# Routing code copied into both branches on the limits, with the flag read before the bias is built

## The chip, the cores and the metric

The kernel runs on one core of a Trainium2 chip. Its time is the device time of one launch in microseconds, and each time given for a kernel is the median of several runs. Engines are TensorE (PE; PEld is its weight load), VectorE (DVE), ScalarE (ACT), GpSimd (POOL) and SyncE (SP), which issues most DMA transfers here. An engine name with a q (PEq, DVEq) is that engine's sequencer, which reads registers, branches and waits.

## The reference

Local attention with a few global keys, then a mixture of 8 experts with one expert per token, then a dense mixture of 4 experts:

```
scores = scale * q @ k.T + bias(n_global, n_local)      # B=2, H=8, S=768, D=64
attn   = softmax(where(keep, scores, -1e9)) @ v         # n_global=8, n_local=96
x      = attn reshaped to [1536, 512]
xn, en = x / |x|, expert_emb / |expert_emb|
logits = xn @ en.T / tau;  idx = argmax(logits);  gate = softmax(logits)[idx]
out    = gate * (relu(x @ w1[idx]) @ w2[idx])           # 8 experts, 512 -> 1024 -> 512
p      = domain_probs / sum
result = sum_e p[:, e] * (relu(out @ v1[e]) @ v2[e])    # 4 experts, all tokens
```

`n_global` and `n_local` are inputs of the program, so the kernel doesn't know them when it is built.

## The kernel before

Each engine runs its own program, and semaphores order them. At the start DVE turns the two limits into a flag `flag_i` (L619 to L625): 1 if the limits are small enough for a windowed attention, 0 if a general one must be used. Every engine but GpSimd reads that flag into a register (`flag_of`, L347) and branches with `If(fast > 0)` ... `Else()`. With the inputs of this case the flag is 1, and the fast branch runs. The general branch is long on DVE and on TensorE (24 unrolled heads and tiles in a loop body), and in the program it lies between the fast branch and what follows both.

In the fast branch attention runs as a pipeline over 4 pairs of heads (`hp`), each with 12 tiles of 128 queries (`i`). `pipeline` writes pair 0 out, loops over pairs 1 and 2, and writes pair 3 out again. For each tile TensorE makes the scores (L1006), DVE adds the bias and takes the row maximum (L703), ACT takes the exponential (L527), TensorE transposes (L1018), ACT copies (L535), TensorE multiplies by the values (L1032), ACT copies (L542), TensorE turns the result (L1046) and DVE normalises it (L738, L740). Beside pair 0 some set-up steps run once: `scale_embeddings` (L643 to L647, of which L645 scales the 8x512 embeddings), `turn_embeddings` on TensorE (L987) and `keep_embeddings` (L654 to L659). `squares` (L680 on DVE, L513 on ACT) sums the squares of each finished tile during the last pair.

Before the pipeline DVE squares the embeddings (L628), waits for the constants (`const_ready`) and builds the bias with six operations (L633 to L638). It reads the flag after these. TensorE runs `keep_busy(32)`, 32 matmuls on a constant tile whose result is never used (L977), waits for the identity matrix (`ident_ready`) and then reads the flag; another `keep_busy(24)` stands between the scores of tile 0 and of tile 1. GpSimd from early on splits weights in two parts (L272 copies the high part, L277 subtracts it for the low part), a quarter of a unit at a time, as the quarters land from DMA.

After the branches comes the routing. On DVE L835 to L887: logits, norms (waiting for `norm_ready` from ACT's root, L519), the maximum, the one-hot table (L849), the ranks that TensorE counts (L1100, L1102), the position of each token (`pos_i`, L866), the tables of slots (up to L881), and the gates (L884 to L887), for which ACT takes one exponential (L561). GpSimd then scatters 12 tiles of tokens to DRAM by `pos_i` (L472). TensorE waits for 8 of them, runs `keep_busy(40)`, and starts the experts with the first gathered tile (L1123); DVE's first step there is L896. The lines that matter most:

```
dve.wait_ge(x_written, HP * DUO)
...
route(nc.vector.tensor_tensor(rt[:, 1], lg[:, 0], lg[:, 1], ALU.add))
...
def flag_of(eng):
    eng.wait_ge(flag_ready, 1)
    return eng.value_load(flag_i[0:1, 0:1], min_val=0, max_val=1)
```

Of the kernel before, what the change touches and what calls it, by code (L numbers as in the profile page):

```python
# [51 lines left out]
def fused_kernel(nc, qkv, limits, emb, tau, probs, wts, consts, out):  # L52
# [6 lines left out]
    with ExitStack() as ctx:  # L59
# [439 lines left out]
        def _(act):  # L499
# [20 lines left out]

            fast = flag_of(act)
            with act.If(fast > 0):
# [23 lines left out]
                norms()  # L546
            with act.Else():
                act.wait_ge(bias_built, 1)
# [60 lines left out]
        def _(dve):  # L609
            done = [0]  # L610

            def step(ins, s=setup_step):
# [14 lines left out]
            dve.wait_ge(emb_ready, 16)  # L627
            nc.vector.tensor_tensor_reduce(out=embq_t, in0=emb_t, in1=emb_t, scale=1.0, scalar=0.0,  # L628
                                           op0=ALU.mult, op1=ALU.add, accum_out=norm_e[:, 0:1]).then_inc(emb_sq, 1)
# [4 lines left out]
            step(nc.vector.scalar_tensor_tensor(mask_t, key_t, ng, mask_t, ALU.is_lt, ALU.max))  # L634
            nc.vector.tensor_scalar(slope_t, rel_t, nl, -0.5 / SCALE, ALU.min, ALU.mult)
            step(nc.vector.tensor_scalar(mask_t, mask_t, -1.0, 64e9 / SCALE, ALU.add, ALU.mult))
            nc.vector.tensor_tensor(bias[:, 0, :], slope_t, mask_t, ALU.add)
            nc.vector.scalar_tensor_tensor(bias[:, 1, :], slope_t, 0.5, mask_t, ALU.mult, ALU.add).then_inc(bias_built, 1)  # L638
            dve.wait_ge(bias_built, 1)
# [9 lines left out]
            def keep_embeddings(idle_times=2):  # L649
# [33 lines left out]

            before_paths = done[0]
            fast = flag_of(dve)
            with dve.If(fast > 0):
                def await_scores(hp, i):


                    n = hp * DUO + i  # L690
                    dve.wait_ge(scores_ready, n + 1)
                    if started(n - 1):
                        dve.wait_ge(transposed, n - 1)
                    if i < 3 and not isinstance(hp, int):
                        dve.wait_ge(bias_ready, 2 * hp if i == 2 else 2 * hp - 1)
# [35 lines left out]
                def normalise(hp, i):  # L731
# [5 lines left out]
                    for hh in range(2):  # L737
# [88 lines left out]
            dve.wait_ge(x_written, HP * DUO)  # L826
            done[0] = 0

            def route(ins):
                step(ins, route_step)  # L830

            def wide(x):
                return x.to_broadcast([P, NT, E])

            route(nc.vector.tensor_tensor(rt[:, 1], lg[:, 0], lg[:, 1], ALU.add))  # L835

            dve.wait_ge(norm_ready, 1)
            route(nc.vector.tensor_scalar(rs[:, 2], rs[:, 1], 1e-6, tau_sb[:, 0:1], ALU.add, ALU.mult))
            route(nc.vector.reciprocal(rs[:, 3], rs[:, 2]))
            route(nc.vector.tensor_tensor(rt[:, 0], rt[:, 1], wide(rs[:, 3]), ALU.mult))  # L840
            route(nc.vector.tensor_reduce(rs[:, 4, :, 0], rt[:, 0], AX.X, ALU.max))
            nc.vector.tensor_tensor(rt[:, 1], rt[:, 0], wide(rs[:, 4]), ALU.subtract).then_inc(shifted_ready, 1)
            dve.wait_ge(shifted_ready, 1)

            route(nc.vector.scalar_tensor_tensor(rt[:, 3], rt[:, 1], 0.0,
                                                 rank8.rearrange("p (a e) -> p a e", a=1).to_broadcast([P, NT, E]),
                                                 ALU.is_ge, ALU.mult))
            route(nc.vector.tensor_reduce(rs[:, 5, :, 0], rt[:, 3], AX.X, ALU.max))
            nc.vector.tensor_tensor(onehot[:, 0:NT, :], rt[:, 3], wide(rs[:, 5]), ALU.is_equal).then_inc(onehot_ready, 1)  # L849


            dve.wait_ge(ranks_ready, 1)
            rank = ps[:, 3, 0:(NT + 1) * E].rearrange("p (t e) -> p t e", e=E)
            route(nc.vector.tensor_scalar(cnt_i[:, 0, :], rank[:, NT, :], float(P - 1), None, ALU.add))
            route(nc.vector.tensor_scalar(cnt_i[:, 1, :], cnt_i[:, 0, :], 7, None, ALU.logical_shift_right))
            route(nc.vector.tensor_scalar(cs[:, 0, :], cnt_i[:, 1, :], 1.0, None, ALU.max))
            slots = cs[:, 0, :].rearrange("p (a f) -> p a f", a=1).to_broadcast([P, E, E])

            route(nc.vector.tensor_tensor(rt[:, 5, 0:E, :], upto[:, 0], slots, ALU.mult))
            route(nc.vector.tensor_reduce(cs[:, 1, :], rt[:, 5, 0:E, :], AX.X, ALU.add))  # L860

# [442 lines left out]
```

## Time and profile before

| | us |
|---|---|
| median of 3 runs | 924.24 (921.68 to 924.5) |
| span of the profiled execution, first to last instruction | 920.3 |
| TensorE matmuls busy | 864.0 (94%) |
| DVE busy | 317.8 (35%) |
| ACT busy | 219.6 (24%) |
| GpSimd busy | 288.0 (31%) |

The page gives no time of the profiled execution but its span. Attention takes the first 135 us or so, the routing and the scatter go to about 165, the 8 experts to about 375, and the dense mixture fills the rest. Engine times are busy times over the span; they say nothing on which of the waits ends last, for which the rows below were read.

### The profile page before, as it was taken

To read this page: it belongs to the slowest core of one execution; us is meant where nothing else is said; L and a number is where in the kernel's file an instruction comes from. 1 tells how busy PE (TensorE), PEld (TensorE's weight loads), DVE (VectorE), ACT (ScalarE), POOL (GpSimd) and SP (SyncE) were. 2 spreads that over 40 slices of the span, in tenths; PEclk is the share of its full clock that TensorE was granted. 3 is DMA by queue.
4 is the path that set the end of the run, shared out by engine and by line. 5 is a ranking of instruction groups with operands and counts; after the bars stand their busy time and mean duration, and the time that the engine had idled before them with its cause. 6 is when DMAs were issued, how large, how long until landed. Compare 5 with 4: busy or idle time off the path is not lost.

```text
span 920.3 us, 12898 instructions
## 1 busy us (share of the span) xinstructions
PE 864.0 (94%) x4433; PEld 697.1 (76%) x4434; DVE 317.8 (35%) x775; ACT 219.6 (24%) x476; POOL 288.0 (31%) x162
## 2 busy tenths in 40 slices
PE   7898862899999999899999999999999999999998
PEld 5566542688887788788888888888888888888886
DVE  7888772344434434122221212121212121212212
ACT  3777580013333333212101111111111111111110
POOL 5363415027778877550000370000740000500000
PEclk9999995999999999999999999999999999999999
DMA  6799643126667766540000140000220000001001
GB/s 243 226 310 308 201 137 138 35 70 210 207 197 228 227 193 194 176 146 1 1 0 0 42 142 0 0 0 0 92 91 1 0 0 0 1 0 46 19 26 46
DMA packets 33075, 90.96 MB, mean 99 GB/s; under 512 B 4232, under 2 KB 4616, under 8 KB 33040
## 3 DMA queue, kind: packets, MB, share of 16 engines
q1 hardware_dynamic: 23056, 54.86, 17.9%
q10 hardware_dynamic: 8064, 29.36, 10.1%
q0 software_dynamic: 1920, 6.29, 2.1%
q8 instruction: 19, 0.31, 0.1%
q14 instruction: 16, 0.13, 0.0%
HBM read 72.67 MB, written 17.83 MB: 98 GB/s over the span
## 4 chain that ended last, share of the span: by engine, by line
PE 81%; DMA 6%; DVE 5%; issue 4%; POOL 1%; ACT 1%; SPq 1%; DVEq 0%; ACTq 0%
PE ps L1207 28%; PE ps L1194 28%; PE ps L1151 10%; PE ps L1133 7%; DMA xg<-x_sorted 3%; PE ps L1018 2%; DMA win<-qkv 1%; PE ps L1006 1%; POOL x_sorted L472 1%; PE ps L1032 1%; PE ps L1141 1%; PE ps L1123 1%; ACT arena L527 1%; PE ps L977 1%; DVE den L722 1%
## 5 line engine op out<-in xcount | busy, mean ns | idle before, releaser
L1207 PE MATMUL ps<-ring,h 128*128 128x512 f32 x1152 | 275.9, 390 | 0.0
L1194 PE MATMUL ps<-ring 128*128 (+1 forms) x864 | 256.4, 389 | 0.0
L277 POOL TENSOR_TENSOR ring<-raw,ring 128x1024 fp32r<-128x1024 f32 x96 | 227.7, 2396 | 83.7 <-ACT ring L272 80.8
L1207 PEld LDWEIGHTS ps<-ring,h 128*128 128x128 f32 x1152 | 215.7, 188 | 44.6
L945 DVE SCALAR_TENSOR_TENSOR h<-ps,h 128x512 fp32r<-128x512 f32 x96 | 66.3, 691 | 366.3 <-ACT h L596 366.3
L1194 PEld LDWEIGHTS ps<-ring 128*128 128x128 f32 x864 | 162.0, 188 | 33.8 <-DVE x2b L938 0.2
L596 ACT ACTIVATE h<-ps 128x512 fp32r<-128x512 f32 x96 | 57.6, 600 | 427.3 <-PE ps L1194 427.3
L272 POOL CAST ring<-raw 128x1024 fp32r<-128x1024 f32 x36 | 37.5, 1043 | 381.5 <-PE ps L1194 321.2
L1194 PE MATMUL ps<-x2b,ring 128*128 (+1 forms) x288 | 112.1, 389 | 0.0
L272 ACT CAST ring<-raw 128x1024 fp32r<-128x1024 f32 x60 | 62.2, 1052 | 176.1 <-PE ps L1151 116.2
L1133 PE MATMUL ps<-ring,xT 128*128 x384 | 91.5, 394 | 0.8 <-DVE xT L898 0.6
L1151 PE MATMUL ps<-ring,hT 128*128 x384 | 91.7, 394 | 0.1
L1133 PEld LDWEIGHTS ps<-ring,xT 128*128 128x128 f32 x384 | 70.9, 188 | 15.4 <-issue 1.3
L1151 PEld LDWEIGHTS ps<-ring,hT 128*128 128x128 f32 x384 | 71.0, 188 | 14.9 <-issue 0.4
L1194 PEld LDWEIGHTS ps<-x2b,ring 128*128 128x128 f32 x288 | 54.1, 188 | 11.2
L527 ACT ACTIVATE arena<-arena,nmax 128x256 f32<-128x256 f32 x96 | 48.0, 501 | 31.5 <-DVE nmax L703 31.4
L1018 PE MATMUL ps<-cst,arena 128*128 128x128 f32 x192 | 31.9, 290 | 16.2 <-ACT arena L527 16.0
L977 PE MATMUL ps<-order_b 128*128 128x256 bf16 x236 | 32.4, 302 | 15.2 <-DMA x_sorted<-xrow,pos_i 14.1
L977 PEld LDWEIGHTS ps<-order_b 128*128 128x128 bf16 x236 | 25.3, 109 | 20.5 <-DMA x_sorted<-xrow,pos_i 14.2
L1018 PEld LDWEIGHTS ps<-cst,arena 128*128 128x128 f32 x192 | 20.4, 142 | 26.3 <-ACT arena L527 22.5
L908 DVE TENSOR_SCALAR hrow<-ps 128x1024 f32<-128x1024 f32 x16 | 19.6, 1226 | 51.9 <-PE ps L1133 51.9
L1006 PE MATMUL ps<-win 64*128 64x256 f32 x192 | 34.1, 432 | 3.5 <-DMA win<-qkv 2.3
(115 smaller groups left out, 528.4 us busy)
## 6 DMA issues: line engine op xcount, KB each, us to landing
raw<-wts ACTq DMA_DIRECT2D x56, 512.0 KB, 4.2
raw<-wts SPq DMA_DIRECT2D x40, 512.0 KB, 3.8
win<-qkv SPq DMA_DIRECT2D x32, 320.0 KB, 4.3
x_sorted<-ring SPq DMA_DIRECT2D x20, 256.0 KB, 5.0
xg<-x_sorted SPq DMA_DIRECT2D x17, 256.0 KB, 3.4
y_sorted<-yrow SPq DMA_DIRECT2D x16, 256.0 KB, 3.9
win<-qkv SPq DMA_DIRECT2D x8, 384.0 KB, 6.1
result<-xrow SPq DMA_DIRECT2D x12, 256.0 KB, 2.1
```

Of the source, the lines that this page charges most:

```text
L272: copy(w_part(u, 0)[:, q * CW:q * CW + CW], raw[:, q, :]).then_inc(high_count(u, q)[0], 1)
L277: nc.gpsimd.tensor_tensor(w_part(u, 1)[:, q * CW:q * CW + CW], raw[:, q, :], w_part(u, 0)[:, q * CW:q * CW + CW].bitcast(F32), ALU.subtrac ...
L527: ins = nc.scalar.activation(pr, pr, ACT.Exp, bias=nmax[:, i % 2, hh:hh + 1], scale=-1.0, accum_out=sums[:, i, hh:hh + 1])
L596: nc.scalar.activation(h2[:, f % 2, 0, :], ps[:, 4 + f % 2, :], ACT.Relu).then_inc(hid_high, 1)
L945: nc.vector.scalar_tensor_tensor(h2[:, f % 2, 1, :], ps[:, 4 + f % 2, :], 0.0, h2[:, f % 2, 0, :].bitcast(F32), ALU.max, ALU.subtract).the ...
L977: ins = nc.tensor.matmul(ps[:, 7, 0:2 * P], order_b[:, 0, :], order_b[:, :, :].rearrange("p n c -> p (n c)"), start=True, stop=True)
L1006: ins = nc.tensor.matmul(ps[:, 2 * (i % 2) + hh, 0:WK], win[r, queries(j, b)], win[r, keys(w, b)], start=True, stop=True)
L1018: ins = nc.tensor.transpose(ps[:, 4 + i % 2, hh * WK + part * P:hh * WK + part * P + P], tb[:, i % 2, hh, c], ident)
L1133: ins = nc.tensor.matmul(ps[:, 1 + half, :], xT[:, xp, k, :], weights(e, 0, wp, k * F + half * 512, 512), start=(k == 0 and n == 0), stop= ...
L1151: ins = nc.tensor.matmul(ps[:, 3, :], hT[:, xp, k, :], weights(e, 1, wp, k * DM, DM), start=(k == 0 and n == 0), stop=(k == KF - 1 and n = ...
L1194: ins = nc.tensor.matmul(ps[:, 4 + f % 2, :], w_part(u1, wp)[:, k * F + f * P:k * F + f * P + P], x2T(xp, k)[:, bass.ds(g * 512, 512)], st ...
L1207: ins = nc.tensor.matmul(ps[:, t, :], h2[:, f % 2, hp_, t * P:t * P + P], w_part(u1 + 1, wp)[:, f * DM:f * DM + DM], start=(f == 0 and n = ...
```

## The change

The routing of DVE becomes a function `route_tokens`, that of TensorE `count_ranks`, and ACT's one exponential `gate_exps`; each is called at the end of both branches, so it stands in the program twice and runs once. On DVE the squares of the embeddings and the bias become functions that are called inside the fast branch, behind the flag read. On TensorE `keep_busy(32)` is split into 8 ahead of the flag read and 24 behind it, and the wait for the identity stands behind these. The bodies of the functions are those of before. The general branch squares the embeddings itself and no longer waits for a bias.

```diff
@@ ACT
+            def gate_exps():
+                act.wait_ge(shifted_ready, 1)
+                nc.scalar.activation(rt[:, 2], rt[:, 1], ACT.Exp).then_inc(exp_ready, 1)
...
                 norms()
+                gate_exps()
             with act.Else():
-                act.wait_ge(bias_built, 1)
...
                 norms()
-            act.wait_ge(shifted_ready, 1)
-            nc.scalar.activation(rt[:, 2], rt[:, 1], ACT.Exp).then_inc(exp_ready, 1)
+                gate_exps()
@@ DVE
-            dve.wait_ge(emb_ready, 16)
-            nc.vector.tensor_tensor_reduce(out=embq_t, in0=emb_t, in1=emb_t, scale=1.0, scalar=0.0,
...
-            dve.wait_ge(const_ready, 16)
-            step(nc.vector.tensor_scalar(mask_t, rel_t, nl, None, ALU.is_lt))
...
+            def square_embeddings():
+                dve.wait_ge(emb_ready, 16)
...
+            def build_bias():
+                dve.wait_ge(const_ready, 16)
+                step(nc.vector.tensor_scalar(mask_t, rel_t, nl, None, ALU.is_lt))
...
-            def keep_embeddings(idle_times=2):
+            def keep_embeddings(idle_times=3):
...
+            def route_tokens():
+                dve.wait_ge(x_written, HP * DUO)
+                done[0] = 0
...
+                route(nc.vector.tensor_tensor(rt[:, 1], lg[:, 0], lg[:, 1], ALU.add))
...
             fast = flag_of(dve)
             with dve.If(fast > 0):
+                square_embeddings()
+                build_bias()
...
                 pipeline(dve, [(await_scores, 0), (denominators, 3), (bias_and_max, 0), (reciprocals, 3),
                                (normalise, 4)],
                          {1: scale_embeddings, 3: keep_embeddings, 6: expert_weights}, {squares: 5})
+                route_tokens()
             with dve.Else():
                 done[0] = before_paths
+                square_embeddings()
...
-            dve.wait_ge(x_written, HP * DUO)
-            done[0] = 0
...
+                route_tokens()
@@ PE
             pe.wait_ge(idle_ready, 1)
-            keep_busy(32)
+            keep_busy(8)
...
-            pe.wait_ge(ident_ready, 16)
+            def count_ranks():
+                pe.wait_ge(x_written, HP * DUO)
+                pe.wait_ge(onehot_ready, 1)
...
             fast = flag_of(pe)
             with pe.If(fast > 0):
+                keep_busy(24)
+                pe.wait_ge(ident_ready, 16)
...
                 pipeline(pe, [(scores, 0), (products, 3), (transposes, 1), (turn, 4)],
                          {0: lambda: keep_busy(24), 2: turn_embeddings})
+                count_ranks()
             with pe.Else():
+                pe.wait_ge(ident_ready, 16)
                 turn_embeddings()
...
-            pe.wait_ge(x_written, HP * DUO)
-            pe.wait_ge(onehot_ready, 1)
...
+                count_ranks()
```

On DVE, this is the end of the fast branch before: the last normalised tile (`lg`, `xrow`), its squares, and the branch over the general path, whose first row is L643.

```order
L738 SCALAR_TENSOR_TENSOR lg<-ps,inv,lg 128x8 x2
L740 TENSOR_TENSOR xrow<-ps,inv 128x128
L680 ISA win,rs<-xrow 128x512
L680 ISA rs 128x1
L686 UNCONDITIONAL_BRANCH
L643 TENSOR_SCALAR norm_e<-norm_e 8x1
```

The branch leads to the end of the general path on DVE, where the routing stands before:

```order
L680 ISA win,rs<-xrow 128x512
L680 ISA rs 128x1
L749 UNCONDITIONAL_BRANCH
L835 TENSOR_TENSOR win<-lg 128x96
L838 TENSOR_SCALAR rs<-rs,tau_sb 128x12
L839 RECIPROCAL rs<-rs 128x12
```

And this is the end of DVE's fast branch now, with the routing's first rows behind the squares (L811 is the old L740, L684 the old L680, L698 the old L835):

```order
L811 TENSOR_TENSOR xrow<-ps,inv 128x128
L684 ISA win,rs<-xrow 128x512
L684 ISA rs 128x1
L698 TENSOR_TENSOR win<-lg 128x96
L701 TENSOR_SCALAR rs<-rs,tau_sb 128x12
L702 RECIPROCAL rs<-rs 128x12
```

No branch lies between the squares and the routing any more; it follows the routing's last row, L750.

TensorE's first rows before, with what each waits for:

```order
L977 MATMUL ps<-order_b 128x256 [waits idle_ready]
L977 MATMUL ps<-order_b 128x256 x31
L347 TENSOR_LOAD flag_i [waits flag_ready,ident_ready]
L347 ISA x2
L993 COMPARE_AND_BRANCH
L1006 MATMUL ps<-win 128x256 [waits win0_ready0]
L1006 MATMUL ps<-win 128x256
L977 MATMUL ps<-order_b 128x256 x24
```

TensorE's first rows now (L988 is the old L977, L1030 the old L1006):

```order
L988 MATMUL ps<-order_b 128x256 [waits idle_ready]
L988 MATMUL ps<-order_b 128x256 x7
L347 TENSOR_LOAD flag_i [waits flag_ready]
L347 ISA x2
L1014 COMPARE_AND_BRANCH
L988 MATMUL ps<-order_b 128x256 x24
L1030 MATMUL ps<-win 128x256 [waits win0_ready0,ident_ready]
L1030 MATMUL ps<-win 128x256
L988 MATMUL ps<-order_b 128x256 x24
```

The flag read moved ahead of 24 of the 32 unused matmuls, and the wait for the identity moved from the flag read to the first scores.

## Rows read from the trace of the kernel before

**Rows 1.** The page, part 4: shares of the chain that ended last, by engine.

```profile
PE 81%; DMA 6%; DVE 5%; issue 4%; POOL 1%; ACT 1%; SPq 1%; DVEq 0%; ACTq 0%
```

**Rows 2.** The chain in order of time, 134.7 to 138.3: start us, us, what.

```profile
134.79 0.02 issue
...
134.88 0.56 issue
...
135.51 2.42 issue
137.93 0.27 DVE win L835
...
138.23 0.24 DVE rs L838
```

**Rows 3.** Timelines of TensorE, GpSimd and DVE, 125 to 172: start, us, instructions [idle before].

```profile
140.61 0.24 PE L1100 MATMUL ps<-onehot,order_b 128*128 128x104 bf16 x1 [7.13 <-DVE onehot L849]
...
155.51 6.46 PE L977 MATMUL ps<-order_b 128*128 128x256 bf16 x40 [14.11 <-DMA x_sorted<-xrow,pos_i]
164.77 0.66 PE L1123 MATMUL ps<-cst,xg 128*128 128x128 f32 x4 [2.80 <-DMA xg<-x_sorted]
...
143.69 1.16 POOL L472 DMA_INDIRECT x_sorted<-xrow,pos_i  x1 [26.08 <-DVE pos_i L866]
...
146.40 0.27 DVE L887 TENSOR_TENSOR dprob<-dprob,rs 128x48 f32<-128x48 f32 x1
165.46 0.69 DVE L896 CAST xT<-ps 128x512 fp32r<-128x512 f32 x1 [18.79 <-PE ps L1123]
```

**Rows 4.** Timeline of ACT at the end of attention.

```profile
135.61 0.21 ACT L519 ACTIVATE rs<-rs 128x12 f32<-128x12 f32 x1 [0.56 <-DVE rs L680]
135.84 1.28 ACT L561 ACT_TABLE_LOAD   x1
139.63 0.28 ACT L561 ACTIVATE win<-win 128x96 f32<-128x96 f32 x1 [2.51 <-DVE win L842]
```

**Rows 5.** Timeline of DVE, 0 to 22.

```profile
3.16 0.15 DVE L625 CAST flag_i<-flag 128x1 int32<-128x1 f32 x1
...
6.03 0.62 DVE L633 TENSOR_SCALAR xrow<-xrow,nf 128x768 f32<-128x768 f32 x1 [2.12 <-DMA xrow<-consts]
...
11.76 0.42 DVE L703 CUSTOM_DVE_ANT_0 arena<-ps,arena 128x256 f32<-128x256 f32 x1 [1.07 <-issue]
...
13.50 2.49 DVE L645 TENSOR_SCALAR xrow<-xrow,norm_e 8x512 f32<-8x512 f32 x1
...
17.14 2.21 DVE L722 TENSOR_SCALAR den<-sums 128x2 f32<-128x2 f32 x1
```

**Rows 6.** Timeline of TensorE, 0 to 22.

```profile
1.11 5.98 PE L977 MATMUL ps<-order_b 128*128 128x256 bf16 x32 [1.11 <-POOL order_b L459]
8.24 0.70 PE L1006 MATMUL ps<-win 64*128 64x256 f32 x4 [1.15 <-issue]
...
11.60 0.70 PE L1006 MATMUL ps<-win 64*128 64x256 f32 x4
```

**Rows 7.** TensorE's flag read at L347: count, ns min/median/max, start.

```profile
L347 PEldq TENSOR_LOAD <-flag_i x1: 496/496/496, 7.2 to 7.2; - x1
```

**Rows 8.** Timeline of GpSimd, 0 to 22.

```profile
13.36 2.36 POOL L277 TENSOR_TENSOR ring<-raw,ring 128x1024 fp32r<-128x1024 f32 x1
```

**Rows 9.** The chain in order of time, 60 to 168: score matmuls of four tiles.

```profile
83.48 0.63 PE ps L1006 x4
...
85.55 0.63 PE ps L1006 x4
...
97.70 0.94 PE ps L1006 x4
...
101.23 0.76 PE ps L1006 x4
```

**Rows 10.** Busy times of PE, PEld, DVE, ACT, POOL, then granted clock, DMA share, GB/s.

```profile
98.00:101.00 3.00, 3.00 (x18) 1.98 (x15) 0.92 (x6) 1.24 (x6) 0.00 (x0) 0.51 0.79 271
```

More of the change, by code:

```diff
@@ L825, in _ @@
                     squares(HP - 1, t)
-            dve.wait_ge(x_written, HP * DUO)
-            done[0] = 0
[L829 to L860, printed above, removed]
-            route(nc.vector.tensor_tensor(rt[:, 0], rank[:, 0:NT, :],
-                                          cs[:, 1, :].rearrange("p (a e) -> p a e", a=1).to_broadcast([P, NT, E]),
-                                          ALU.add))
@@ L865, in _ @@
-            route(nc.vector.tensor_tensor(rt[:, 4], rt[:, 0], onehot[:, 0:NT, :], ALU.mult))
-            nc.vector.tensor_reduce(pos_i[:, :], rt[:, 4], AX.X, ALU.max).then_inc(pos_ready, 1)
-            route(nc.vector.tensor_tensor(rt[:, 5, 0:E, :], upto[:, 1], slots, ALU.mult))
-            route(nc.vector.tensor_reduce(cs[:, 2, :], rt[:, 5, 0:E, :], AX.X, ALU.add))
-            route(nc.vector.tensor_tensor(own[:, :, :],
-                                          cs[:, 2, :].rearrange("p (a e) -> p a e", a=1).to_broadcast([P, MAXS, E]),
-                                          slotno.rearrange("p (s a) -> p s a", a=1).to_broadcast([P, MAXS, E]),
-                                          ALU.is_le))
@@ L989, in turn_embeddings @@
                 ins.then_inc(embT_ready, 1)
-            pe.wait_ge(ident_ready, 16)
+            def count_ranks():
+                pe.wait_ge(x_written, HP * DUO)
+                pe.wait_ge(onehot_ready, 1)
+                oh = onehot[:, :, :].rearrange("p t e -> p (t e)")
+                end = (NT + 1) * E
+                nc.tensor.matmul(ps[:, 3, 0:end], order_b[:, 0, :], oh, start=True, stop=False).then_inc(slots_done, 1)
+                for n in range(1, NT + 1):
+                    ins = nc.tensor.matmul(ps[:, 3, n * E:end], order_b[:, 1, :], oh[:, 0:end - n * E], start=False,
+                                           stop=(n == NT))
+                ins.then_inc(ranks_ready, 1)
             fast = flag_of(pe)
             with pe.If(fast > 0):
+                keep_busy(24)
+                pe.wait_ge(ident_ready, 16)
                 def scores(hp, i):
@@ L1093, in _ @@
                                              start=True, stop=True).then_inc(g_logits, 1)
-            pe.wait_ge(x_written, HP * DUO)
-            pe.wait_ge(onehot_ready, 1)
-            oh = onehot[:, :, :].rearrange("p t e -> p (t e)")
-            end = (NT + 1) * E
-            nc.tensor.matmul(ps[:, 3, 0:end], order_b[:, 0, :], oh, start=True, stop=False).then_inc(slots_done, 1)
-            for n in range(1, NT + 1):
-                ins = nc.tensor.matmul(ps[:, 3, n * E:end], order_b[:, 1, :], oh[:, 0:end - n * E], start=False,
-                                       stop=(n == NT))
-            ins.then_inc(ranks_ready, 1)
+                count_ranks()
             pe.wait_ge(tables_ready, 1)
```

72 lines of the change are left out of this document (54 added, 18 removed).

## Prediction

> **What bounds the kernel now.** I read the page first, for the shares of the chain that ended last: TensorE's matmuls are 81% of it, DVE 5%, "issue" (time in which the engine waited for nothing that the profile shows) 4% [rows 1]. So most of the span is dense expert matmuls that this change does not touch, and what it can win must lie in the small items. I then read the chain in order of time where attention ends and the routing begins, because the routing is what moves. The reader sees there that DVE's part of the chain is in "issue" from 134.88, behind the start of its last squares (L680) and with the jump over the other branch (L686) next in its program, and that it starts the first routing instruction, L835, only at 137.93 [rows 2]. Of that, 2.42 us stand bare on the chain. Next the timeline of the engines that wait for the routing: TensorE has idled 7.13 us for the one-hot table, GpSimd starts the scatter at 143.69, released by `pos_i`, TensorE's warming matmuls start when scattered tiles have landed, and the first expert tile comes at 164.77 [rows 3]. Nothing there waits for weights, so a shift of the routing passes whole into the expert part, and from there to the end, where TensorE leads. Last I read the first 20 us, engine by engine, for the other half of the change.
>
> **Part 1: the routing stands in the branch.** Before, DVE jumps over the long other branch to L835. After, L698 (the old L835) follows the squares directly (order rows). Straight neighbours on DVE leave hardly a gap: 0.02 us behind L740, and L838 starts 0.30 us after L835, whose own time is 0.27 [rows 2]. So L698 should start at about 135.54. The next instruction needs `norm_ready`, which ACT sets when the root at L519 ends: 135.61 + 0.21 = 135.82, and a hand-over of up to 0.1 us (DVE's squares end at 135.51, ACT's root starts at 135.61) gives about 135.9 for the old L838 [rows 2, 4]. It was at 138.23. The saving is 138.23 - 135.9 = **2.33 us**. Its upper bound is the bare 2.42; its lower bound 0, if straight code at that place has to be fetched as well. I take the upper region, since the squares and products just ahead, also straight code, show gaps of 0.02.
>
> The Trainium skill ("Runtime: NRT & Kernel Launch", section "Instruction fetch mechanics") says that a taken branch to code outside a small window of blocks forces a fetch before execution goes on, while straight code is fetched ahead. The one bare wait of rows 2 agrees; by the rule the whole of it goes, as in my sum.
>
> The jump isn't gone, it now stands behind the routing. DVE meets it at 146.67 - 2.33 = 144.3 and has nothing to do until the first expert tile, for which it idles 18.79 us [rows 3]; 3.05 us (134.88 to 137.93) of jump are covered six times. TensorE's jump moves behind the rank matmuls, which begin at 140.61 - 2.33 and take 0.8: 139.1 + 3.05 = 142.2, and it then idles until 155.51 - 2.33 [rows 3]. ACT's jump moves behind its exp, now at about 137.3; its next copy waits for expert slots. The exp itself needs a table load that ends at 137.12, and its input comes at about 137.27 (139.63 - 2.33), so it still fits, by 0.15 us, and nobody on the chain waits for it [rows 4]. If that cover failed, the exp would be late by tenths and only the last four DVE operations would notice. The copies of code cost nothing else: the same instructions run once.
>
> **Part 2: the flag is read early.** DVE's flag read and branch, 1.07 us of idle time between the bias (which ends at 11.76 - 1.07 = 10.69) and the first L703 at 11.76, move into the time when DVE waited for the constants anyway (2.12 us idle before 6.03) [rows 5]. So the first L703 can start at 10.7. Does that pass on? The second tile's scores need TensorE. There the order is now 8 warming matmuls, flag read, 24 warming matmuls, scores of tile 0, 24 more, scores of tile 1. The flag is set at 3.31 [rows 5]; TensorE's read took from 7.2 to the first score matmul at 8.24, so 1.04 [rows 6, 7]. The 24 therefore start at about 4.4. Their pace has two ends: 24 ran between the two score pairs in 11.60 - 8.24 - 0.70 = 2.66 us at full clock, twice that, 5.3, at half. The 32 of the start took 5.98, 0.187 each, a mix [rows 6]. Scores of tile 0 thus start between 7.2 (when the flag read that waits for the identity began [rows 7]) and 9.7; since TensorE has done only 8 matmuls and then stood for 1.5 us, I take the slow end, **9.5**, against 8.24 before. So TensorE gets later by 1.3 us where DVE gets earlier by 1.07.
>
> What does the later tile 1 cost? Before, L645 (scaling the embeddings) was ready 5.26 us after the start of tile 0's scores (13.50 - 8.24), and then took 2.49 us for an 8x512 operation: GpSimd's subtraction, started at 13.36, ended at 15.72, and L645 ended at 15.99 [rows 5, 6, 8]. It was held until GpSimd was through. In the new order it is ready at about 9.5 + 5.26 = 14.8, still before 15.72, and ends at 15.99 again. From there every engine stands where it stood. The start is worth **0**, with the cover being GpSimd's operation: it holds for a start of tile 0's scores between 8.1 (13.36 - 5.26) and 10.5 (15.72 - 5.26). Below 8.1 L645 slips in ahead and saves up to 2.2 us (2.49 less some 0.3, by the 0.27 of the nearest small operation, L835 [rows 2]); above 10.5 the delay shows. If TensorE also ran the second 24 and the two score pairs at half clock, each would take twice as long, 2.66 + 2 x 0.70 = 4.1 us more: 9.7 + 5.26 + 4.1 = 19.0, a loss of up to 3.3 (19.0 - 15.72).
>
> The Trainium skill ("SBUF — State Buffer", section on the ports of the engines and their practical consequences) says that a DVE tensor_scalar in a two-port mode and a GpSimd operation lock a shared pair of ports, and the first to issue blocks the other. L645's 2.49 us agree. The other page that bears here, "TensorE: Matmul & The Clock Gate", says TensorE starts at half clock and rises only after sustained work, so breaking the warm-up after 8 matmuls speaks against the change; it would put the scores of tile 0 near 9.5, inside the cover above, or past it if the rise is late (rival D).
>
> **The sum.** Span 920.3 - 2.33 + 0 = 917.97. The page gives only the span; the median of the runs, 924.24, lies 3.94 above it, which I take to be what lies around the span. 917.97 + 3.94 = **921.9**, 0.25% faster.
>
> **The rivals.**
> A, the forecast: 2.33 at the join, 0 at the start: 921.9, chance 0.50; its own range 920.8 to 923.0, from a spread of runs of 2.8 us.
> B, the start pays too: the clock rises early, tile 0's scores start under 8.1, L645 goes ahead of GpSimd, or DVE's 1.07 passes on by another way. For: before, L645 missed by 0.14 us only (13.50 against 13.36). Against: the later score pair, and the next small operation, L722 at 17.14, was held 2.21 us in the same way, so a gain can be lost there [rows 5]. 1.07 to 2.2 more: 920.8 to 919.7. Chance 0.17.
> C, it doesn't do what it says: the straight routing code has to be fetched as well, and the 2.42 stay: 924.2. Against it, the 0.02 gaps ahead. Chance 0.10.
> D, TensorE's broken warm-up outlasts GpSimd's cover and eats 1 to 3.3 us: 922.9 to 925.2. Chance 0.12.
> E, slower: TensorE's clock stays at half into the tiles of attention. A tile at half clock took 101.23 - 97.70 = 3.53 us, at full 85.55 - 83.48 = 2.07, so 1.46 each [rows 9, 10]. To lose 0.3% in all it must cost 2.33 + 2.8 = 5.1, that is from four tiles on; four cost 5.8: 927.7. Against: at 98.0 to 101 a granted clock of 0.51 was back within about two tiles. Chance 0.06. The remaining 0.05 is for what I don't see, on either side.
>
> **How the numbers follow.** About 0.3% (2.8 us) is what a measurement of this kernel can tell from no change. The forecast's 2.33 lies just under that bound, so of A's 0.50 some 0.19 falls beyond it; with B's 0.17 and 0.01 of the rest, faster is 0.37. Same is A's other 0.31, C 0.10, D 0.12, 0.01 of the rest: 0.54. Slower: E and 0.03: 0.09. The range reaches from B's far end to past C and D: 919.5 to 924.8; it leaves out E, and the edges of B and D.
>
> **What would show it.** Right: L698 starts within 0.1 us of the last squares; the next row waits for ACT's root; `pos_i` to scatter, to first expert tile as before; L649 (the old L645) ends at about 16.0 whatever its start; TensorE's first scores start near 9.5. Wrong: an "issue" gap of 1 us or more ahead of or inside the routing (C); L649 taking 0.3 us and DVE ahead from 16 us on (B); L649 ready past 15.7 (D); a granted clock of 0.5 in the tiles behind 16 us (E). The prediction would also be wrong if attention's later waits for windows, which chain the rest of it to DMA, fell out otherwise though its start is the same.

## The result, and the profile after

The changed kernel takes 915.21 us (median of 9 runs, 913.62 to 920.15), the kernel before 921.68 (median of 9, 916.99 to 924.5). The ratio is 0.9937, 95% interval [0.9918, 0.9957]: 0.4 to 0.8% faster. 921.9 was predicted, which is 6.7 us above the measured time. The profiled execution of the changed kernel was its longest run: 920.15 us, of which the span is 918.3. So its span must not be set against the 920.3 of before; the stages inside it can be.

The page, part 4, the shares of the chain that ended last, answers to [rows 1] and shows nothing new:

```profile
PE 82%; DMA 6%; DVE 4%; issue 4%; POOL 1%; ACT 1%; SPq 0%; DVEq 0%; ACTq 0%
```

The chain where attention ends and the routing begins (start us, us, what), which answers to [rows 2]:

```profile
137.91 0.02 DVE rs L684
137.93 0.02 issue
...
138.01 0.22 ACT rs L519
...
138.33 0.24 DVE rs L701
138.57 0.02 issue
138.60 0.24 DVE rs L702
```

The bare 2.42 us of "issue" are gone. The squares (L684) end at 137.93 on the chain (137.91 on DVE's timeline, which the joins below go by); ACT's root follows, and L701 (the old L838) starts at 138.33, 0.40 us behind the squares, where it took 2.72 (138.23 - 135.51) before. The timelines of TensorE, GpSimd, DVE and ACT behind it, which answer to [rows 3] and [rows 4]:

```profile
140.72 0.25 PE L1007 MATMUL ps<-onehot,order_b 128*128 128x104 bf16 x1 [4.83 <-DVE onehot L712]
...
155.62 7.00 PE L988 MATMUL ps<-order_b 128*128 128x256 bf16 x40 [14.12 <-DMA x_sorted<-xrow,pos_i]
163.62 0.66 PE L1138 MATMUL ps<-cst,xg 128*128 128x128 f32 x4 [1.00 <-DMA xg<-x_sorted]
...
143.80 1.16 POOL L472 DMA_INDIRECT x_sorted<-xrow,pos_i  x1 [23.85 <-DVE pos_i L729]
...
164.31 0.69 DVE L907 CAST xT<-ps 128x512 fp32r<-128x512 f32 x1 [17.53 <-PE ps L1138]
...
138.24 1.28 ACT L523 ACT_TABLE_LOAD   x1
139.73 0.28 ACT L523 ACTIVATE win<-win 128x96 f32<-128x96 f32 x1 [0.21 <-DVE win L705]
```

From the last squares to the first scatter it is 5.89 us (143.80 - 137.91), against 8.18 (143.69 - 135.51) before. DVE's and TensorE's jumps lie in idle times of 17.53 and 14.12 us, and ACT's table is loaded 0.21 us before its input comes.

But there is a second difference, which the prediction doesn't have. TensorE had stood still for 2.80 us ahead of the first expert tile [rows 3]; here it is 1.00. The chain of the changed kernel there:

```profile
157.93 2.90 DMA x_sorted<-xrow,pos_i
...
160.90 2.67 DMA xg<-x_sorted
163.57 0.04 issue
163.62 0.66 PE ps L1138 x4
```

And that of the kernel before:

```profile
157.82 4.22 DMA x_sorted<-xrow,pos_i
...
162.12 2.61 DMA xg<-x_sorted
164.73 0.04 issue
164.77 0.66 PE ps L1123 x4
```

The last scatter is issued at nearly the same time in both (157.82 and 157.93), but it lands after 2.90 us instead of 4.22.

The start, by the timelines of TensorE, DVE and GpSimd, which answer to [rows 5, 6, 8]:

```profile
1.11 1.89 PE L988 MATMUL ps<-order_b 128*128 128x256 bf16 x8 [1.11 <-POOL order_b L459]
4.36 4.11 PE L988 MATMUL ps<-order_b 128*128 128x256 bf16 x24 [1.36 <-issue]
8.40 0.70 PE L1030 MATMUL ps<-win 64*128 64x256 f32 x4
...
10.56 0.43 DVE L774 CUSTOM_DVE_ANT_0 arena<-ps,arena 128x256 f32<-128x256 f32 x1
...
12.51 0.42 DVE L774 CUSTOM_DVE_ANT_0 arena<-ps,arena 128x256 f32<-128x256 f32 x1 [1.17 <-PE ps L1030]
...
13.56 2.55 DVE L649 TENSOR_SCALAR xrow<-xrow,norm_e 8x512 f32<-8x512 f32 x1
...
17.25 2.22 DVE L793 TENSOR_SCALAR den<-sums 128x2 f32<-128x2 f32 x1
...
13.48 2.35 POOL L277 TENSOR_TENSOR ring<-raw,ring 128x1024 fp32r<-128x1024 f32 x1
```

DVE's first maximum comes 1.20 us earlier than at 11.76, waits 1.17 us for TensorE's second scores, and L649 (the old L645) then again sits beside GpSimd's subtraction and ends at 16.11 (before: 15.99). From there on all is as before.

### The profile page after: what moved, and what is told of

Its sections match the earlier page's. It is cut to its first block, busy times and chain, and to the rows that moved or that the text cites. A ratio compares the mean times of both kernels' runs of the same rounds, so it can differ in the third digit from the quotient of the medians.

```text
span 918.3 us, 12897 instructions
## 1 busy us (share of the span) xinstructions
PE 867.8 (95%) x4433; PEld 698.5 (76%) x4434; DVE 319.4 (35%) x775; ACT 220.6 (24%) x476; POOL 287.9 (31%) x162
## 4 chain that ended last, share of the span: by engine, by line
PE 82%; DMA 6%; DVE 4%; issue 4%; POOL 1%; ACT 1%; SPq 0%; DVEq 0%; ACTq 0%
PE ps L1222 28%; PE ps L1209 28%; PE ps L1166 10%; PE ps L1148 7%; DMA xg<-x_sorted 3%; PE ps L1042 2%; PE ps L1030 2%; PE ps L988 1%; PE ps L1056 1%; DMA win<-qkv 1%; POOL x_sorted L472 1%; PE ps L1156 1%; PE ps L1138 1%; ACT arena L531 1%; DVE arena L774 1%
## 5 line engine op out<-in xcount | busy, mean ns | idle before, releaser
L988 PE MATMUL ps<-order_b 128*128 128x256 bf16 x236 | 32.2, 300 | 16.6 <-DMA x_sorted<-xrow,pos_i 14.1
L988 PEld LDWEIGHTS ps<-order_b 128*128 128x128 bf16 x236 | 24.8, 107 | 22.2 <-DMA x_sorted<-xrow,pos_i 14.2
L774 DVE CUSTOM_DVE_ANT_0 arena<-ps,arena 128x256 f32<-128x256 f32 x96 | 36.5, 416 | 1.3 <-PE ps L1030 1.2
```

The costliest lines, as they stand in the source:

```text
L774: ins = nc.vector.tensor_tensor_reduce(out=tb[:, i % 2, hh, :], in0=ps[:, 2 * (i % 2) + hh, 0:WK], in1=bias[:, hh, v:v + WK], scale=-SCALE ...
L988: ins = nc.tensor.matmul(ps[:, 7, 0:2 * P], order_b[:, 0, :], order_b[:, :, :].rearrange("p n c -> p (n c)"), start=True, stop=True)
```

## The experiments

I took the same segments from each profile. "Join" is the end of the last squares to the first scatter's issue; "tile" the last scatter's issue to the first expert transposes; "gather" the start of TensorE's `keep_busy(72)` ahead of the dense mixture to its first transposes; "rest" from there to the end of the span. "Code" counts the matmuls by which TensorE's code behind the branches lies further on than in the kernel before. "Packet" tells where the 16 KB packet of instructions begins that falls nearest the last scatter's issue, in us from that issue: the number is the start of the 0.25 us step in which it begins, so +0.25 stands for +0.25 to +0.50. Ratios are to the kernel before on the same chip.

| kernel | code | join | packet | tile | gather | rest | ratio |
|---|---|---|---|---|---|---|---|
| before | 0 | 8.18 | +0.25 | 6.95 | 10.00 | 536.8 | |
| again_before | 0 | 7.90 | +0.25 | 7.03 | 9.22 | 536.2 | 0.9991 [0.9975, 1.0008] |
| before_third | 0 | 7.91 | +0.25 | 6.95 | 9.17 | 536.3 | 1.0007 [0.9990, 1.0024] |
| front_only | 0 | 7.90 | +0.25 | 6.52 | 9.10 | 536.3 | 0.9977 [0.9960, 0.9994] |
| flag_dve * | 0 | 7.90 | +0.25 | 6.60 | 9.67 | 538.7 | 0.9992 [0.9973, 1.0012] |
| act30 | 0 | 8.14 | +0.25 | 6.61 | 9.24 | 535.9 | 0.9998 [0.9980, 1.0017] |
| dve30 | 0 | 8.09 | +0.25 | 6.35 | 9.38 | 536.2 | 0.9981 [0.9965, 0.9997] |
| route_dve * | 0 | 5.88 | +0.25 | 6.71 | 8.44 | 542.5 | 0.9992 [0.9970, 1.0013] |
| route_dve_again * | 0 | 5.89 | +0.25 | 6.82 | 8.97 | 544.0 | 0.9966 [0.9946, 0.9986] |
| pad13 * | 13 | 7.94 | -1.25 | 5.43 | 8.98 | 541.9 | 1.0044 [1.0023, 1.0064] |
| pad13_again | 13 | 8.10 | -1.25 | 5.47 | 8.84 | 536.5 | 0.9972 [0.9958, 0.9986] |
| pe_ranks * | 13 | 7.93 | -1.25 | 5.36 | 7.95 | 542.8 | 0.9986 [0.9967, 1.0006] |
| pe_ranks_again | 13 | 7.90 | -1.50 | 5.65 | 9.05 | 536.3 | 0.9966 [0.9947, 0.9986] |
| route_only | 13 | 5.87 | -1.25 | 5.95 | 8.36 | 536.2 | 0.9939 [0.9917, 0.9961] |
| after | 13 | 5.89 | -1.25 | 5.69 | 8.73 | 536.4 | 0.9937 [0.9918, 0.9957] |
| again_after | 13 | 5.87 | -1.50 | 5.45 | 8.82 | 536.4 | 0.9927 [0.9898, 0.9955] |
| after_third | 13 | 5.88 | -1.25 | 5.80 | 8.65 | 536.3 | 0.9949 [0.9928, 0.9971] |
| after_pad13 | 26 | 5.88 | -9.25 | 5.46 | 8.23 | 536.4 | 0.9923 [0.9899, 0.9947] |
| pad40 * | 40 | 8.04 | -10.50 | 5.38 | 7.87 | 546.4 | 1.0065 [1.0047, 1.0083] |
| pad40_again * | 40 | 7.91 | -10.50 | 5.45 | 7.87 | 544.5 | 1.0005 [0.9982, 1.0027] |

The runs behind the first pair came in five groups, each on one chip with the kernel before beside it. The star marks the kernels of two of these groups; what is different there is told under "The same code on another chip".

### The two kernels again, and the change in two parts

**again_before and again_after** are the two kernels unchanged.

> The kernel before, unchanged, to see how its time and the length of attention spread from execution to execution. If attention has one length, its profile shows the last squares ending near 135.5 us and the ratio is 1.000 within 0.3%. If it has several (theory 'spread': waits for windows and TensorE's clock fall out otherwise in each execution), the end of attention moves by 2 us or more while everything behind it is unchanged.

> The changed kernel once more. Its first profiled execution was its longest, 920.15 us, with attention 2.5 us longer than before. Theory 'join and start': a typical execution has attention ending at 131 to 133.5 us, the routing 0.5 us behind it, ratio 0.993 to 0.996. Theory 'join alone': attention ends at 135.5 as before, ratio 0.9975.

**route_only** has the routing in both branches and the start of the kernel before; **front_only** the reverse. Against the changed kernel, route_only's diff is

```
-            keep_busy(8)
+            keep_busy(32)
...
-                keep_busy(24)
-                pe.wait_ge(ident_ready, 16)
...
+            square_embeddings()
+            build_bias()
             before_paths = done[0]
             fast = flag_of(dve)
             with dve.If(fast > 0):
-                square_embeddings()
-                build_bias()
```

and front_only's, here for DVE (ACT's exponential and TensorE's ranks go the same way):

```
                          {1: scale_embeddings, 3: keep_embeddings, 6: expert_weights}, {squares: 5})
-                route_tokens()
...
                     squares(HP - 1, t)
-                route_tokens()
+            route_tokens()
```

> Only the routing in the branches; the start as before. Theory 'join alone' and theory 'join and start' both say 2.1 to 2.4 us faster, 0.9975, and a gap of under 0.6 us ahead of the routing. If the whole 6 us come from here, there must be a second thing that the new place of the code saves.

> Only the early flag and the split warming matmuls; the routing behind both branches as before. Theory 'join and start': 3 to 4.5 us faster, 0.995 to 0.997, with attention ending earlier. Theory 'start absorbed' (as predicted): same within 0.15%, the 2.4 us gap ahead of the routing still there.

again_after gave 0.9927, so the gain is real and larger than 2.33 us. route_only has all of it at 0.9939; front_only has little (0.9977), and the join of before. So the gain comes with the routing. But the join, 2.0 to 2.3 us shorter in each profile that has the routing in DVE's branch, is only some 40% of it.

### Where TensorE's code lies

**pad13 and pad40** are the kernel before with 13 (or 40) matmuls that are never executed:

```
             with pe.Else():
+                keep_busy(13)
                 turn_embeddings()
```

The rank count has 13 matmuls (1 + 12, the rows of L1007 and L1009), so with a copy in each branch all of TensorE's later code lies as far on as with `keep_busy(13)`. pad40 has `keep_busy(40)` at the same place.

> The kernel before with 13 matmuls more in the general branch, which never run; they move TensorE's later code by as much as the rank count does in the changed kernel. Theory 'code position': the 16 KB instruction fetch that now runs beside the last scatter and beside the last store of the experts moves out of their way; the last scatter lands 2.7 to 3.2 us after its issue and not 4.2, the last store 4.0 and not 4.4 to 5.2; in all 1 to 2.5 us faster, 0.997 to 0.999. Rival 'only the join pays': nothing that runs has changed, ratio 1.000.

> The same with 40 matmuls that never run. Theory 'code position': the fetch moves three times as far, by 8 us at TensorE's slow pace, to before the warming matmuls at the scatter; the last scatter lands after 2.7 to 3.2 us; at the last store the fetch comes earlier, too, or another takes its place. Ratio 0.997 to 1.000. Rival: 1.000.

In pad13 the join is that of before, and the first expert tile still comes 1.5 us earlier. The page's list of DMA queues has two that carry instructions: q8, in 19 packets of 16 KB in both kernels, and q14, in 16 and 18 packets that are mostly of 8 KB. This section is about q8. What the DMA engines moved from 158.0 to 158.5 in the kernel before, just behind the last scatter's issue at 157.82 (queue, kind, packets, MB, share of 16 engines):

```profile
q0 software_dynamic: 40, 0.16, 85.0%
q8 instruction: 1, 0.02, 22.0%
```

And in the changed kernel from 156.6 to 157.1, ahead of the last issue at 157.93:

```profile
q0 software_dynamic: 17, 0.07, 35.8%
q8 instruction: 1, 0.02, 15.9%
```

The one instruction packet holds a DMA engine for 22.0% of 16 x 0.5 = 1.8 us (1.3 in the changed kernel), in the middle of the scatter's small packets (q0, 0.16 MB in 40). A scatter has landed when its last packet has. With the packet 0.25 to 0.5 us behind the last issue, all nine profiles have tiles of 6.35 to 7.03 us; with it over 1 us ahead or further off, all eleven have 5.36 to 5.95, whatever else the kernels do. The trace keeps each packet's start and length, and they bind the two more closely: in the nine profiles the packet ends 1.66 to 2.19 us behind the last issue, and the first expert tile begins 4.7 to 4.9 us behind the packet's end in every one of them, so the spread of these nine tiles is almost wholly the packet's. The packet's place goes with TensorE's code alone: moving DVE's or ACT's left it at +0.25 (next section).

The later landing costs a second time in some executions. TensorE is out of filler matmuls and stands. Its timeline in before_third, which is the kernel before unchanged:

```profile
155.59 6.25 PE L977 MATMUL ps<-order_b 128*128 128x256 bf16 x40 [14.09 <-DMA x_sorted<-xrow,pos_i]
164.82 0.66 PE L1123 MATMUL ps<-cst,xg 128*128 128x128 f32 x4 [2.98 <-DMA xg<-x_sorted]
165.31 2.99 PE L977 MATMUL ps<-order_b 128*128 128x256 bf16 x16
```

and its windows (us, busy time of PE, PEld, DVE, ACT and POOL, granted clock, DMA share, GB/s):

```profile
162.00:164.00 2.00, 0.00 (x0) 0.00 (x0) 0.00 (x0) 0.00 (x0) 0.00 (x0) 1.00 0.32 80
164.00:166.00 2.00, 1.18 (x11) 1.10 (x12) 0.49 (x1) 0.00 (x0) 0.00 (x0) 0.99 0.14 51
166.00:168.00 2.00, 2.00 (x13) 1.45 (x10) 0.89 (x2) 0.00 (x0) 0.00 (x0) 0.50 0.52 131
```

After 2.98 us of standing the granted clock fell to 0.50 (1.2 GHz) behind the first tile, and the 16 filler matmuls took 2.99 us. In the first profile of the kernel before TensorE stood 2.80 us, kept 1.00 (2.4 GHz), and the same 16 took 1.91. The three profiles in which it stood 2.98 us or more (again_before, before_third and flag_dve) lost 1.2 us so (9.4 instead of 8.1 to 8.2 us from the first expert tile to the second); the other six with the packet at +0.25, and all eleven with it elsewhere, did not.

### The second halves: DVE's and ACT's part, and the flag

**route_dve** copies the routing on DVE and ACT alone, with the start of the kernel before; TensorE's `count_ranks()` stays behind the branches, and its code where it was. **flag_dve** reads the flag early on DVE alone; TensorE's start and the routing are those of before. In TensorE's part both differ from the changed kernel by this, beside the restored start:

```
                          {0: lambda: keep_busy(24), 2: turn_embeddings})
-                count_ranks()
...
-                count_ranks()
+            count_ranks()
```

> The routing in the branches on DVE and ACT, but TensorE's rank count behind both, so TensorE's later code lies where it lay before. Theory 'code position': the join still pays its 2.0 to 2.4 us, but the last scatter takes 3.9 to 4.3 us to land as before; 0.9975 and so 1.5 to 3 us slower than with all of the routing moved. Rival 'only the join pays': as fast as with all of the routing moved, 0.994.

> Only DVE's early flag, with the bias in the branch; TensorE's start and the routing as before. Theory 'start absorbed': DVE's first maximum starts 1.1 us earlier, the third tile's denominators end with GpSimd's second subtraction as before, same within 0.15%. Rival 'the start pays by another way': 0.998, as was measured for both halves of the start together.

route_dve has the short join (5.88) with the packet at +0.25 and the long tile (6.71): so the join belongs to DVE's copy and the tile to TensorE's place, each without the other. flag_dve shortens none of these segments. Neither ratio shows a gain (0.9992 both, on a starred chip).

**pe_ranks**, later, is the other half: only TensorE's count in both branches. Three kernels were run with it or after it a second time: **pad13, route_dve and pad40**. pe_ranks against the kernel before:

```
+                count_ranks()
             with pe.Else():
...
-            pe.wait_ge(x_written, HP * DUO)
-            pe.wait_ge(onehot_ready, 1)
...
+                count_ranks()
```

> TensorE's counting of ranks copied into both branches, VectorE's and ScalarE's routing behind them as before: the other half. The join keeps its 7.9 to 8.1 us, since the wait ahead of the first addition is VectorE's. If TensorE's code places are worth 2 to 2.6 us, this half alone has them: first tile 5.4 to 5.9 us behind the last scatter's issue, ratio 0.996 to 0.998. If they bring nothing and the 13 matmuls' 0.9972 was a chance, 0.999 to 1.001. Together with the other half it should give the change's 0.993 to 0.994 if the two add up.

> TensorE's counting of ranks alone copied into both branches, a second time. Join 7.9 to 8.1 us, first tile 5.4 us behind the last scatter's issue. Ratio 0.9965 to 0.998 in a submission without the stall (its code places then are worth 2 to 2.6 us), 0.998 to 1.000 where the stall shows in its profile.

> The kernel before with 13 matmuls, never run, at the head of TensorE's Else: the same edit as in the run before with 13, a second time. It tells whether the late ScalarE copy at the start of the dense part (4.4 us in that profile) belongs to the code's places or to one execution. Places: the same stall of 3.5 to 5 us ahead of the last of the four x2 copies, last scatter landing in about 3 us, first expert tile 5.4 us behind the last scatter's issue, ratio 1.002 to 1.006. One execution's chance: no stall in this profile and rest of the run at 536.3 us, ratio nearer 0.998, since only the earlier first tile (1.2 us) and the earlier gather (0.8 us) are left.

> The routing copied into both branches on VectorE and ScalarE alone, TensorE's counting of ranks behind them as before: the same edit a second time, in another submission. If the stall of 4 to 6 us at the start of the dense part in its first profile belonged to that submission, it is gone here, and what is left is the join's 2.1 us: ratio 0.997 to 0.9985, first tile still 6.5 to 7 us behind the last scatter's issue. If the stall is this kernel's, it is there again and the ratio is 0.999 to 1.002.

pe_ranks keeps the join (7.93, 7.90) and has the short tile. Its second run gave 0.9966 and pad13's second 0.9972: on those two chips the place of TensorE's code alone is worth 0.14 to 0.53% by the one interval and 0.14 to 0.42% by the other, without one executed instruction changed in pad13. (Their first runs, 0.9986 and 1.0044, fell on the two chips of the starred groups.)

**dve30 and act30** move DVE's (shown) and ACT's later code by 30 instructions that are never executed; **after_pad13** moves TensorE's in the changed kernel by another 13.

```
             with dve.Else():
+                for _ in range(30):
+                    nc.vector.tensor_copy(rs[:, 0], rs[:, 1])
```

> The kernel before with 30 small copies, never run, at the head of VectorE's Else, so that VectorE's code behind the branches lies 30 instructions further on, about as in the changed kernel, and TensorE's where it was. If only TensorE's code matters, everything stays: ratio 0.999 to 1.001, first tile 6.5 to 7 us behind the last scatter's issue, no stall at the start of the dense part. If VectorE's place is what brought the stall where the routing stood in the branches on VectorE and ScalarE alone, a stall of 4 to 6 us stands ahead of TensorE's first dense matmul and the ratio is 1.002 to 1.006.

> The kernel before with 30 small copies, never run, at the head of ScalarE's Else. The stalls at the start of the dense part began at a ScalarE copy whose transposes were done; if ScalarE was out of instructions there, moving its code by 30 should bring such a stall to the kernel before, or move a wait of some us to another ScalarE instruction: ratio 1.002 or more, with idle time that no other engine explains ahead of a ScalarE instruction. If ScalarE's code has no part in it: 0.999 to 1.001 and segments as before.

> The changed kernel with 13 matmuls, never run, at the head of TensorE's Else. The join's 2.1 us stay in every theory (5.9 us from the last squares to the first scatter). If the rest of the change's gain, 3.5 us behind the join in the medians, is the change's own doing, the ratio stays at 0.993 to 0.994. If it is where TensorE's code lies (the 16 KB instruction packet beside the last scatter), the shift by another 13 matmuls moves the packet again: still off the scatter as with 40 (first tile 5.4 to 5.9 us behind its issue), and what then decides is whether the dense part's start stalls: with a stall of 4 to 6 us, 0.998 to 1.000; without one, 0.993.

Neither moved the packet or brought a stall. act30 is level. dve30's 0.9981 lies just under 1, though its segments are those of before. 0.4 us of it can be found outside the segments, in the time of an execution less its span. Where VectorE's program is that of the kernel before, this is 2.14 to 2.29 us in all 249 executions; where it is changed, be it by dve30's never-executed copies, by the early flag or by the routing, it is 1.75 to 2.01 us in all 101, the changed kernel's among them (1.81 on average). So VectorE's code has a part of its own in the gain; why it shortens the time around the span stays open, and so does the rest of dve30's 0.9981. after_pad13 stays at 0.9923: the packet is off the scatter there too.

### The same code on another chip

pad13 gave 1.0044 and, on another chip, 0.9972. The intervals exclude each other, so the first was not this code's doing alone. ScalarE's timeline in pad13, at the four copies that begin the dense mixture:

```profile
378.25 0.59 ACT L586 CAST ring<-ps 128x512 fp32r<-128x512 f32 x1 [3.80 <-PE ps L1179]
379.80 0.59 ACT L586 CAST ring<-ps 128x512 fp32r<-128x512 f32 x1 [0.97 <-issue]
381.52 0.59 ACT L586 CAST ring<-ps 128x512 fp32r<-128x512 f32 x1 [1.13 <-PE ps L1179]
386.48 0.59 ACT L586 CAST ring<-ps 128x512 fp32r<-128x512 f32 x1 [4.37 <-issue]
```

And the last two in pad13_again:

```profile
388.35 0.59 ACT L586 CAST ring<-ps 128x512 fp32r<-128x512 f32 x1 [0.85 <-PE ps L1179]
389.79 0.59 ACT L586 CAST ring<-ps 128x512 fp32r<-128x512 f32 x1 [0.86 <-PE ps L1179]
```

In pad13 TensorE's transposes for the last copy had ended at 382.52, yet ACT starts it at 386.48; DVE and TensorE wait behind it. Such a wait with complete inputs is called the stall here. Six of the seven starred profiles have such a wait at these copies. In the seventh (flag_dve) it stands one step later: ScalarE's first hidden tile begins 7.00 us behind TensorE's first matmul of the dense mixture (386.80 to 393.80), against 3.06 in route_only. Their rest is 538.7 to 546.4 us. None of the thirteen others has such a wait (535.9 to 536.8).

> The kernel before with 40 matmuls, never run, in TensorE's Else, a second time, in another submission. If its 1.0065 was that submission's stall, the stall (8.8 us ahead of TensorE's first dense matmul) is gone, the first tile lies 5.4 us behind the last scatter's issue and the ratio is 0.996 to 0.999. If the stall is made by where the code lies, it is there again and the ratio is 1.004 to 1.008.

> The kernel before, unchanged. Ratio 0.998 to 1.002. If the stall at the start of the dense part belongs to a submission and not to a kernel, this profile has it where the two beside it have it (rest 538 to 546 us) and has none where they have none (536.2 us).

> The changed kernel, unchanged. Where no stall occurs in this submission, 0.992 to 0.995 as before. Where it occurs in all profiles alike, the same 0.992 to 0.996; if the changed code lay so that it met the stall more than the kernel before does, as the padded kernels did, 0.997 to 1.000.

pad40_again fell on such a chip too, and has the stall again, but the ratio 1.0005 instead of 1.0065. before_third and after_third ran on a chip without it, so neither the kernel before nor the changed one was profiled beside the stall, and the changed kernel's time on such a chip was not measured. On the two chips that show it the kernel before had medians of 924.66 and 925.72 us, elsewhere 921.68 to 922.77, so it probably loses something there as well, but less than pad13 did.

## Why the prediction was wrong

**Part 1 (the join) was right.** L698 follows the squares at once, L701 starts 0.40 us behind them (predicted 0.39), and the join is 2.29 us shorter in the first pair of profiles, 2.03 in the two others; 2.33 was predicted. route_dve and route_dve_again show it alone. Rival C falls: straight code at that place comes without a gap. That the jump waits for instructions can be seen as well. What the DMA engines moved from 136.0 to 136.5 in the kernel before, behind the squares' end at 135.51:

```profile
q14 instruction: 1, 0.01, 3.8%
```

All thirteen profiles in which DVE jumps there have such an 8 KB packet 0.31 to 0.59 us behind the squares, and L835 starts 1.4 to 1.5 us after its end; the seven with straight code have none within 2 us of the squares, and no such wait. In the first profile of before the packet began 0.59 us behind the squares and in again_before and before_third 0.32 and 0.31, which is why its jump took 2.42 us and theirs 2.14.

The jumps behind the routing are covered by the waits that were named, and ACT's exponential fits by 0.21 us (predicted 0.15). (The prediction's 3.05 us for a jump counts from the start of the last squares and so holds their own time too; behind them it is 2.42.)

**The step that failed is the sentence "The copies of code cost nothing else: the same instructions run once", and with it the sum.** The copies do change something though they run once: they move all of TensorE's later code by 13 matmuls, and with it the moment at which its next 16 KB of instructions are fetched. What the sum lacked, from the three pairs of profiles:

- the first expert tile: mean 6.98 before, 5.65 after, **1.33 us**;
- the half clock behind it: 1.2 us in two of three profiles of before, in three of the nine with that code place, in none after: about **0.4**;
- the gather ahead of the dense mixture: mean 9.46 before, 8.73 after, **0.7**. The last store of expert results lands in 4.4 to 5.2 us before and in 3.8 to 4.1 after. pad13's two profiles, with nothing changed but the place of TensorE's code, have 8.98 and 8.84, so most of it goes with that place. That it is the packet beside the store, as at the scatter, was not isolated;
- the time around the span: 2.2 us before, 1.8 after, **0.4**, which goes with VectorE's code (dve30 shows it alone).

The Trainium skill ("Runtime: NRT & Kernel Launch", section "Instruction fetch mechanics") says that crossing a block of instructions costs one bump of a queue and is mostly hidden. For the engine that fetches, the trace agrees: TensorE waits for no instructions there. What wasn't hidden here is the packet's time on a DMA engine that others were waiting for, the 1.33 us of the first item.

With the join's 2.1 the four items make 4.9 us, 0.53%. The three measured ratios mean 0.9938, 5.7 us. 4.9 lies inside all three intervals; some 0.8 us has no place in this account. Attention's end varies from 131.5 to 138.0 us between executions, so a us there can't be seen in single profiles. That stays open.

**Part 2 (the start) was right in its result.** Worth 0: route_only (0.9939) equals the changed kernel (0.9937, 0.9927, 0.9949). The cover, GpSimd's subtraction, did what was said: L649 was ready at 13.56 in the first profile and at 14.42 in after_third, and ended at 16.11 and at 15.97. The cover held the other way as well: in route_dve, route_dve_again and pe_ranks, which have the start of before, that instruction got in ahead of the subtraction and took 0.47 to 0.60 us instead of 2.49, yet DVE's second L722 behind it still began at 21.10 to 21.33, as in the first profile of before (21.12). Only in pad13, where GpSimd began later (14.09), did it come earlier (18.31). TensorE's 24 matmuls took 4.11 us, between the two bounds, and the first scores came at 8.40 (after_third 9.26, again_after 9.50; 9.5 predicted, so in the first profile it was 1.1 us out, but inside the cover). Rival D falls. Against rival B stand the profiles and route_only against the changed kernel; for it stands front_only's 0.9977, whose interval leaves out 1. 0.3 us of its 2 lie around the span (1.91 us on average, against 2.21), and its join and its start show no gain over the kernel before. The rest I leave unexplained, so B is unlikely but not refuted. The granted clock did fall to 0.67 and then 0.50 from 17 to 24 us in the changed kernel's first profile, but in after_third it fell from 26 to 29 us (0.50), as in before_third, whose start is untouched (0.50 from 26 to 32), and in again_after not at all up to 35 us. The fall from 17 to 24 us stands in that one profile alone, and the change as a whole gained, so rival E didn't come about.

**The base was high.** The sum was made against 924.24, a median of 3, and took 3.94 us for what lies around the span. In every other execution whose span is known it is 1.75 to 2.29 us, and nine runs of the kernel before have the median 921.68. So of the 6.7 us between 921.9 and 915.2, 2.6 are the base (924.24 - 921.68) and 4.1 are what the sum lacked. The base alone would have put the forecast at 919.4, and the measured time still 4.1 us under it.

**What follows for the chances.** "Same" was put at 0.54 since 2.33 us lies under what can be told. The trace of before held a sign that the prediction didn't read: ten of the twelve scatters landed 2.70 to 2.91 us after their issue, and the last two after 3.78 and 4.22. Which way the packet would move was not known in advance, but that moving code can move it, and is worth over a us, should have widened the range below 919.5.

## What to carry to other kernels

Code that is copied, padded or moved on one engine shifts that engine's later instruction fetches. A 16 KB packet that fell on a transfer for which TensorE waited cost 1.3 us in this kernel, and another 1.2 in the executions in which TensorE's clock then fell. Before crediting an edit with a small gain, run the kernel before with never-executed instructions of the same number at the same place, and compare the segments of the profiles, not the total. DVE's jump over the long other branch cost 2.1 to 2.4 us bare here; it was free once it stood where its engine waits anyway.

## What the runs showed of the hardware that was not expected

- The same kernel stood at 1.0044 [1.0023, 1.0064] of the kernel before on one chip and at 0.9972 [0.9958, 0.9986] on another. What goes with it in the profiles is a wait of ScalarE of some 4 us or more for which no input is missing, near one place of the program. In five of the seven profiles with such a wait no instruction packet lies inside it; in route_dve and route_dve_again one of 8 KB (q14) does, but the changed kernel has one at the same place (386.48 us) without a wait. So the cause stays open, and that ScalarE lacks instructions there was not shown.
- The moment of the 16 KB packet is reproducible to a quarter of a us: it begins 0.35 to 0.50 us behind the last scatter's issue in nine profiles of six different kernels, and 1.05 to 1.29 us ahead of it in eight profiles of four.
- Never-executed instructions on VectorE shortened the time around the span by 0.4 us (dve30, 1.76 to 1.86 us in its twelve executions; 2.14 to 2.29 with the unchanged program).
